# Attention with split operands: who rounds the turned queries and keys, who takes their rests, and when queries and keys are turned

## The reference, cut to what matters

```
scores = scale * q @ k.T                      # q, k, v: [4, 8, 576, 64] float32
thresh = max(scores, -1) - tau                # keep scores >= thresh, else -1e9
attn = softmax(scores);  x = attn @ v         # [2304, 512]
logits = x @ w_gate + modality_bias[id]       # top-1 of 8 experts, gate = its softmax
x = gate * (relu(x @ w1[e]) @ w2[e])          # w1 [8, 512, 1024]
h = x @ w_in;  out = (h * sigmoid(1.702 h)) @ w_out
```

## Time and profile before

| | us |
|---|---|
| median of 3 runs (lowest, highest) | 1011.82 (1011.54, 1012.12) |
| profiled execution, its own time | 1011.9 |
| its span | 1010.3 |
| PE / DVE / ACT / POOL busy | 967.1 / 530.6 / 432.4 / 286.2 |

### The profile page before, as it was taken

The page is one execution under the profiler, slowest core; times in us unless marked ns, Lnnn a source line. Parts: engine busy times, 40 slices in busy tenths (PEclk is TensorE's granted clock), DMA queues, the critical chain, the costliest instruction groups (busy, mean ns, idle before and its releaser), DMA issues.

```text
span 1010.3 us, 18677 instructions
## 1 busy us (share of the span) xinstructions
PE 967.1 (96%) x6365; PEld 853.6 (84%) x6366; DVE 530.6 (53%) x1138; ACT 432.4 (43%) x925; POOL 286.2 (28%) x357
## 2 busy tenths in 40 slices
PE   4999999999998899999999999999999999999996
PEld 4777777777676699999999999989999999999995
DVE  5998888999999875411124245522223223222221
ACT  3777787776667713312114254432222222222221
POOL 4766667676666503211112100010010000100101
PEclk8999999999999999999999999999999999999999
DMA  4334343334351506711110633110100100100000
GB/s 88 79 82 94 89 97 91 89 78 91 81 158 45 161 13 208 231 42 42 47 57 21 229 107 101 46 60 1 32 31 0 39 23 23 39 0 0 32 1 32
DMA packets 110669, 70.23 MB, mean 70 GB/s; under 512 B 87161, under 2 KB 95383, under 8 KB 110615
## 3 DMA queue, kind: packets, MB, share of 16 engines
q1 hardware_dynamic: 99959, 53.51, 20.3%
q0 software_dynamic: 4160, 10.51, 3.3%
q10 hardware_dynamic: 6496, 5.54, 1.7%
HBM read 45.68 MB, written 14.70 MB: 60 GB/s over the span
## 4 chain that ended last, share of the span: by engine, by line
PE 76%; DVE 12%; issue 7%; ACT 3%; DVEq 1%; DMA 0%; ACTq 0%; POOL 0%; POOLq 0%
PE s_ps L1842 19%; PE s_ps L1814 13%; PE s_ps L1687 11%; PE pt_ps L1814 6%; DVE probs L835 6%; PE misc L1762 5%; PE o_ps L1762 5%; PE s_ps L1620 5%; PE o_ps L1634 5%; PE pt_ps L1570 4%; DVE scores L1124 2%; ACT probs L1427 1%; PE pt_ps L1679 1%; PE pt_ps L1565 1%; DVE xs L844 1%
## 5 line engine op out<-in xcount | busy, mean ns | idle before, releaser
L1312 DVE TENSOR_TENSOR g<-s_ps,sig 128x384 f32<-128x384 f32 x96 | 53.5, 558 | 277.1 <-ACT sig L1537 277.1
L1537 ACT ACTIVATE sig<-s_ps 128x384 f32<-128x384 f32 x96 | 47.2, 491 | 271.5 <-PE s_ps L1842 271.5
L835 DVE SCALAR_TENSOR_TENSOR probs<-scores,thresh,probs 128x576 f32<-128x576 f32 x144 | 158.5, 1102 | 0.0
L790 POOL DMA_INDIRECT out_dram<-out_sb,table x18 | 17.8, 989 | 417.7 <-ACT out_sb L1512 414.7
L1124 DVE TENSOR_SCALAR_CACHE_REDUCE scores<-s_ps,taus 128x576 f32<-128x576 f32 x144 | 117.6, 817 | 31.2 <-PE s_ps L1620 11.4
L1427 ACT ACTIVATE probs<-scores,row_low 128x576 f32<-128x576 f32 x144 | 113.0, 785 | 45.4 <-DVE scores L1124 44.3
L1570 PE MATMUL pt_ps<-ident,probs 128*128 128x128 f32 x720 | 121.9, 280 | 10.7 <-ACT pT L1335 6.6
L1842 PE MATMUL s_ps<-yT_high,w_in_high 128*128 (+1 forms) x384 | 129.6, 337 | 0.3 <-issue 0.2
L1842 PE MATMUL s_ps<-yT_high,w_in_low 128*128 (+1 forms) x384 | 129.6, 338 | 0.0
L1842 PE MATMUL s_ps<-yT_low,w_in_high 128*128 (+1 forms) x384 | 129.1, 336 | 0.0
L1570 PEld LDWEIGHTS pt_ps<-ident,probs 128*128 128x128 f32 x720 | 83.3, 142 | 41.5 <-issue 25.5
(11 more groups left out here) (273 smaller groups left out, 2221.0 us busy)
## 6 DMA issues: line engine op xcount, KB each, us to landing
w_raw<-in_moe_w_dram SPq DMA_DIRECT2D x24, 512.0 KB, 4.5
yT_dram<-tile_yT ACTq DMA_DIRECT2D x10, 512.0 KB, 3.1
k_parts<-k_swap SPq DMA_DIRECT2D x31, 144.0 KB, 2.3
k_swap<-k_parts SPq DMA_DIRECT2D x31, 144.0 KB, 2.3
x_dram<-xs SPq DMA_DIRECT2D x32, 128.0 KB, 2.3
w_in_raw<-in_moe_w_in_dram SPq DMA_DIRECT2D x4, 1024.0 KB, 5.2
w_out_raw<-in_moe_w_out_dram SPq DMA_DIRECT2D x16, 256.0 KB, 2.7
qk<-in_k_dram SPq DMA_DIRECT2D x30, 128.0 KB, 2.4
```

Of the source, the lines that this page charges most:

```text
L835: dve.scalar_tensor_tensor(out=probs[:, i % PROB_SLOTS, 0:SEQ], in0=scores[:, i % SCORE_SLOTS], scalar=thresh[:, j, u:u + 1], in1=probs[:, ...
```

## The change

- GpSimd keeps only the threshold. ScalarE rounds: `round_both` (128 x 576: queries into the top of `q_parts`, keys into its bottom for a while) and `round_keys` (64 x 576 into the bottom of `k_swap`), side 0 after passes 3 and 4, side 1 after passes 5 and 7.
- VectorE takes both rests in one operation (`split_rests`, 128 x 576), in pass 4 after `write_x` (side 0) and in pass 7 (side 1). The rests land in `k_parts`, so the rest of the queries is in the wrong place.
- SyncE moves three things per side instead of two: the queries' rest and the keys' rest (`move_rests`), and, once the first has landed, the rounded keys (`move_keys`).
- SyncE's order in a pair p is now `move_rests` side 1 of p, `load_b` of p+2, `move_keys` side 1, `load_v`, `move_rests` side 0 of p+1, `store_x` of p-2, `move_keys` side 0, `load_a` of p+2.
- The nine tiles are turned in passes 0 to 4, two each but one in pass 2; TensorE waits for `load_b` in pass 3.
- The expert identifiers are loaded in pairs 2 to 5, not in the opening, and the bias of the rows is taken in quad 4. One early gather of rows moves from step 13 of the last quad to step 3.

```diff
-        TURN_TILES = {1: (0, 2), 3: (2, 4), 4: (4, 5), 6: (5, 7), 8: (7, 9)}
+        TURN_TILES = [(0, 2), (2, 4), (4, 5), (5, 7), (7, 9)]
@@ SyncE, load_a and load_b
-                    wait_apart(sp, turned, (quad * 2 + j - 1) * U)
+                    wait_apart(sp, turned, U if isinstance(quad, int) and quad * 2 + j == 2 else (quad * 2 + j - 2) * U + TPB)
-            def swap_keys(quad, j, side):
...
+            def move_rests(quad, j, side):
+                cols = K_COLS[side]
+                wait_apart(sp, split_low, (quad * 2 + j) * 2 + side)
+                sp.dma_start(q_parts[j][BOTTOM, Q_COLS[side]].bitcast(F32), k_parts[j][TOP, cols].bitcast(F32)
+                             ).then_inc(q_moved[side], 16)
+                sp.dma_start(k_swap[j][TOP, cols].bitcast(F32), k_parts[j][BOTTOM, cols].bitcast(F32)).then_inc(k_swapped[side], 16)
+            def move_keys(quad, j, side):
+                cols, pair = K_COLS[side], quad * 2 + j
+                wait_apart(sp, split_high, (pair * 2 + side) * 2)
+                wait_apart(sp, q_moved[side], (pair + side) * 16)
                 sp.dma_start(k_parts[j][TOP, cols].bitcast(F32), k_swap[j][BOTTOM, cols].bitcast(F32)).then_inc(k_swapped[side], 16)
@@ SyncE, step
+                    if on(pair, 1, PAIRS):
+                        move_rests(quad, j, 1)
                     if on(pair, 0, PAIRS - 2):
                         load_b(quad + 1, j)
-                    if on(pair, 0, PAIRS):
-                        swap_keys(quad, j, 1)
+                    if on(pair, 1, PAIRS):
+                        move_keys(quad, j, 1)
...
                     if on(pair, 0, PAIRS):
                         load_v(quad, j)
+                    if on(pair, 0, PAIRS - 1):
+                        move_rests(quad + j, 1 - j, 0)
+                    if on(pair, 2, PAIRS + 2):
+                        store_x(quad - 1, j)
+                    if on(pair, 0, PAIRS - 1):
+                        move_keys(quad + j, 1 - j, 0)
+                    if w1_pass:
+                        load_w1(first_expert_of(sp), 0, range(2, DB))
                     if on(pair, 0, PAIRS - 2):
                         load_a(quad + 1, j)
-                    if on(pair, 0, PAIRS - 1):
-                        swap_keys(quad + j, 1 - j, 0)
...
+                    if quad in (1, 2):
+                        load_ids(quad - 1, j)
@@ SyncE, opening: after load_b(0, 1)
+            move_rests(0, 0, 1)
             sp.dma_start(bias_sb[:], ...
...
-            for bp in range(BATCH // 2):        # eight loads of ids
...
+            move_keys(0, 0, 1)
             step(0)
@@ VectorE
+            def split_rests(pair, j, side):
+                cols = K_COLS[side]
+                wait(dve, split_high, (pair * 2 + side) * 2 - 1)
+                dve.tensor_tensor(k_parts[j][:, cols], qkT_raw[:, cols], q_parts[j][:, Q_COLS[side]].bitcast(F32), ALU.subtract
+                                  ).then_inc(split_low, 1)
...
+                    if u in (4, 7) and on(pair, 0, PAIRS - 1):
+                        split_rests(pair + 1, 1 - j, 0 if u == 4 else 1)
                     if on(n, 2, UNITS + 2):
                         mask(n - 2, (i - 2) % STEPS)
@@ ScalarE
+            def round_both(j, side):
+                act.copy(q_parts[j][:, Q_COLS[side]], qkT_raw[:, K_COLS[side]]).then_inc(split_high, 1)
+            def round_keys(j, side):
+                act.copy(k_swap[j][BOTTOM, K_COLS[side]], qkT_raw[BOTTOM, K_COLS[side]]).then_inc(split_high, 1)
...
+                    if u in (3, 4, 5, 7) and on(pair, 0, PAIRS - 1):
+                        side = 0 if u < 5 else 1
+                        if u in (3, 5):
+                            wait_apart(act, turned_copied, pair * U + U + (TAIL - 1 if side == 0 else TPB))
+                            round_both(1 - j, side)
+                        else:
+                            round_keys(1 - j, side)
@@ TensorE
-                if with_qk and tu in (0, TPB):
+                if with_qk and tu in (0, 3):
                     loaded, each = (qk_a_loaded, A_LOADS) if tu == 0 else (qk_b_loaded, B_LOADS)
                     wait(pe, loaded[1 - j], (quad + 1 + j) * each)
...
-                if with_qk:
-                    mm = transpose_qk(1 - j, tu, pt_ps[:, QK_AT + TURN_SLOT[tu]])
+                if with_qk and tu < TPB:
+                    first, end = TURN_TILES[tu]
+                    for tile in range(first, end):
+                        mm = transpose_qk(1 - j, tile, pt_ps[:, QK_AT + tile - first])
```

More of the change, by code:

```diff
@@ L285, in attention_moe_mlp_kernel @@
         k_swapped = [sem(f"k_swapped{side}") for side in range(2)]
+        q_moved = [sem(f"q_moved{side}") for side in range(2)]
         first_copied = sem("first_copied")
@@ L294, in attention_moe_mlp_kernel @@
         tau_ready = sem("tau_ready")
-        parts_ready = sem("parts_ready")
+        split_high = sem("split_high")
+        split_low = sem("split_low")
         scores_ready = sem("scores_ready")
@@ L414, in attention_moe_mlp_kernel @@
         TOP, BOTTOM = slice(0, DH), slice(DH, P)
-        TURN_SLOT = [0, 1] * (TPB // 2) + [0] + [0, 1] * (TAIL // 2)
-        TURN_TILES = {1: (0, 2), 3: (2, 4), 4: (4, 5), 6: (5, 7), 8: (7, 9)}
+        TURN_TILES = [(0, 2), (2, 4), (4, 5), (5, 7), (7, 9)]
         assert TPB == 5
@@ L480, in load_b @@
                              ).then_inc(qk_b_loaded[j], 16)
-            def swap_keys(quad, j, side):
-                split = (quad * 2 + j) * 8 + side * 4 - 4
+            def move_rests(quad, j, side):
                 cols = K_COLS[side]
-                wait_apart(sp, parts_ready, split + 1)
+                wait_apart(sp, split_low, (quad * 2 + j) * 2 + side)
[6 more added lines that the diff above has]
+                wait_apart(sp, q_moved[side], (pair + side) * 16)
                 sp.dma_start(k_parts[j][TOP, cols].bitcast(F32), k_swap[j][BOTTOM, cols].bitcast(F32)).then_inc(k_swapped[side], 16)
-                wait_apart(sp, parts_ready, split + 2)
-                sp.dma_start(k_swap[j][TOP, cols].bitcast(F32), k_parts[j][BOTTOM, cols].bitcast(F32)).then_inc(k_swapped[side], 16)
             def load_v(quad, j):
@@ L566, in early_part, with load_ids @@
                     sp.wait_ge(turned, UNITS)
-                    sp.wait_ge(parts_ready, PAIRS * 8 - 4)
+                    sp.wait_ge(split_high, (PAIRS * 2 - 1) * 2)
+                    sp.wait_ge(split_low, PAIRS * 2 - 1)
                     sp.wait_ge(order_stored, 16)
                     load_w2(first_expert_of(sp), 0)
+            def load_ids(bp, part):
+                at = bp * U
+                id_words = modality_id.bitcast(I32).rearrange("(b s w) -> b s w", b=BATCH, w=2)[:, :, 0]
+                ids_of = id_words[2 * bp + part]
+                rows, tail, cols = ((slice(0, LAST), SEQ - LAST, slice(at, at + TAIL)) if part == 0 else
+                                    (slice(LAST, P), SEQ - LAST, slice(at + TPB, at + U)))
+                sp.dma_start(ids[:, cols], ids_of[0:SEQ - LAST].rearrange("(t p) -> p t", p=P),
+                             allow_slow_non_contiguous=True).then_inc(routing_loaded, 16)
+                sp.dma_start(ids[rows, at + TAIL:at + TPB], ids_of[tail:].rearrange("(t p) -> p t", t=1),
+                             allow_slow_non_contiguous=True).then_inc(routing_loaded, 16)
             def first_expert_of(sp):
@@ L577, in step @@
                     pair = quad * 2 + j
+                    w1_pass = isinstance(quad, int) and (quad, j) == (QUADS - 2, 1)
+                    if on(pair, 1, PAIRS):
+                        move_rests(quad, j, 1)
                     if on(pair, 0, PAIRS - 2):
                         load_b(quad + 1, j)
-                    if on(pair, 0, PAIRS):
-                        swap_keys(quad, j, 1)
+                    if on(pair, 1, PAIRS):
+                        move_keys(quad, j, 1)
                     if isinstance(quad, int):
                         early_part(quad, j)
-                    if isinstance(quad, int) and (quad, j) == (QUADS - 2, 1):
+                    if w1_pass:
                         sp.wait_ge(first_expert_ready, 1)
@@ L612, in _ @@
                              w_gate.rearrange("(h p) e -> p h e", p=DH)).then_inc(gate_loaded, 16)
-            id_words = modality_id.bitcast(I32).rearrange("(b s w) -> b s w", b=BATCH, w=2)[:, :, 0]
-            for bp in range(BATCH // 2):
[L615 to L624, removed]
+            move_keys(0, 0, 1)
             step(0)
@@ L678, in _ @@
         def _(pool):
[L679 to L698, removed]
             pool.memset(ident[:], 0.0).then_inc(consts, 1)
@@ L719, in _ @@
                                pattern=[[1, P]], channel_multiplier=-1).then_inc(routing_consts, 1)
-            pool.wait_ge(routing_consts, 9)
-            split_keys(0, 0, 1)
-            split_queries(0, 0, 1)
             pool.wait_ge(tau_ready, 5)
@@ L736, in step @@
```

(25 more changed lines are left out.)

## The result

The changed kernel takes 1046.0 us (median of 4, 1041.8 to 1047.7) against 1011.9: a ratio of 1.033, 95% interval 1.031 to 1.035. It is slower, as forecast, but by 34 us and not by 16, and it lies outside the range. Its profiled execution took 1041.8, with a span of 1040.2 against 1010.3.

What follows compares the result with a forecast made beforehand. TensorE's own pace was taken to bound the loop (19.41 us a pair), with VectorE weighing most in later quads. Shifts from -3.5 in pair 0 to +17.8 at V(14), then +15.9, gave 1011.9 + 15.9 = 1028 us, range 1002 to 1040.

Steps and rivals of the forecast that it cites:

- Opening: Pair 0: with the identifiers' eight loads no longer ahead, TensorE resumes at 17.1 instead of 21.55, 4.5 us early.
- S: End of VectorE's rest in pass 4, which SyncE's moves, stores and loads wait for; 162.7 in pair 7's clock.
- V(1): First value matmul of pair 1, V(p) being that of pair p; forecast to shift by -3.5 us against before.
- The split's prices: ScalarE's rounding 0.67 us, VectorE's rest 0.75, its mask 0.82 instead of 1.05 in the loop and 1.14 later.
- The late load: Loop: load_a's sixth load lands 9.2 us behind S, 2.6 late for pass 0; period 21.7 us instead of 19.4.
- X to S: From pass 0's turning to the end of VectorE's rest in pass 4: 10.4 us of TensorE plus 2.0 of VectorE.
- the w1 term: Pair 13: two 512 KB loads of w1 stand ahead of load_a, +2.5 us, bounds 1 and 6.
- The tail: V(14) to attention's end: nothing more is loaded, VectorE is relieved by 1.4, then 0.5 us; shift +17.8 becomes +15.9.
- A: Rival: load_a is not on the path, TensorE keeps 19.4 us in the loop, later quads gain; 996 us, chance 0.13.
- B: Rival: as A, but ScalarE's roundings cost 0.5 us in each of seven loop periods; 1003 us, chance 0.06.
- C: Rival: SyncE's queue is crowded, the sixth load takes 0.9 us more in each of 13 periods; 1040 us, chance 0.15.
- D: Rival: GpSimd's threshold still stretches the mask, the load is only partly late, gain and loss cancel; 1012 us, chance 0.06.

## Why the prediction was wrong

- **Opening.** Forecast: TensorE resumes at 17.1. Measured: 17.14. X(1), pass 0 of pair 1, was forecast at 28.9 and came at 28.6. That is right partly by luck, as two errors cancel: the eight scores ran at the higher clock and S came at 19.97 instead of 20.9, and from S to X(1) took 8.7 instead of 8.0. V(1) came at 32.9 and not at 31.4, because the clock had fallen behind the stall.
- **The split's prices.** Forecast: rounding 0.67, rest 0.75, mask back at 0.82. Groups of the changed kernel, 60 to 200 us (busy, mean ns, idle before):
```profile
L1345 ACT CAST q_parts<-qkT_raw 128x576 fp32r<-128x576 f32 x12 | 8.2, 682 | 0.0
...
L815 DVE TENSOR_TENSOR k_parts<-qkT_raw,q_parts 128x576 fp32r<-128x576 f32 x12 | 9.0, 751 | 0.0
L824 DVE SCALAR_TENSOR_TENSOR probs<-scores,thresh,probs 128x576 f32<-128x576 f32 x54 | 43.9, 813 | 0.0
```
- **The late load.** Forecast: S to pass 0 is 9.3 us, the load 2.6 us late. Measured: 9.36 in pair 7, 9.5 on average over pairs 2 to 8, stalls mostly of 1.8 to 2.5. Right, and shown by moving load_a back, which takes away 46 us, the clock's share included.
- **X to S, the step that failed.** I put 12.4 us from pass 0's turning (X) to VectorE's rest (S), and took TensorE's 10.4 of it from a trace in which it never stood still. The cost of the lower clock behind a stall stood at nothing. In pair 5, where the clock did not fall, the sum comes out: from 120.83 to the end of this rest is 12.45 us.
```profile
132.53 0.75 DVE L815 TENSOR_TENSOR k_parts<-qkT_raw,q_parts 128x576 fp32r<-128x576 f32 x1
```
The four other pairs without a fall take 12.3 to 12.5. In pair 7, where it fell, it is 166.49 to 180.53, 14.0; the nine pairs with a fall take 13.8 to 15.2, together 16 us more than 9 x 12.4. So the whole miss of this step is the clock. I had seen the opening at half pace (0.44 a score matmul) and allowed for it there, but gave none of the 14 stalls that I forecast this consequence. The filled stall prices it at 15.3 us. With it the forecast of +16 would have been +31; 34 were measured.
- **What else was off.** Between V(2) and V(8) the changed kernel loses 23.2 us where 13.8 were forecast. Of the 9.4 more, 7.8 lie behind an X and are the lower clock, and 1.6 lie between S and X, which took 9.6 us on average and not 9.3. So even at the higher clock the period is not 21.7: from X(5) to X(6) it is 21.9, and 22.2 in the run with the stalls filled. V(13) to V(14) is 26.1, but 1.6 of it is the lower clock; the 24.5 that are left agree with the forecast 22.1 + 2.5, so the w1 term held. The tail gained more: V(14) to V(16) is 38.7 against 44.2, 5.5 us less where 1.9 were forecast; VectorE's relief was undersized (in V(14) to V(15) the mask took 1.21 us on average before and takes 0.81 now, and I had used 1.14). The tail pulls against the rest.
- **The rivals.** A was the mechanism of the unchanged order: it gave 996, and the kernel with load_a early takes 1000.3, 994.2 once ScalarE's rounding is moved. B was half right: with load_a early, ScalarE's rounding in pass 7 costs 0.3 us a period (19.8 against 19.5; not in passes 3 and 4, where I put it), but behind the late load it is hidden. C does not explain the miss: in the stalls of pairs 1 to 9 the sixth load landed in 1.9 to 2.2, and only two of the 14 took longer, 3.0 and 3.1. D is refuted: the mask is at 0.81 and the load fully late.
- **The range** reached 1040 by crowding of the queue alone. A stall on TensorE had to carry the lower clock as a term of its own, with both ends (0 and 14 x 1.6 = 22 us, by the price that pair 7 shows), and the range would have held the result.

What stays open: why the clock falls after one stall of about 2 us and not after the next. The traces show both, and no run here tells them apart.

## What to carry to other kernels

When an engine takes over work, follow the order of the queue that moves its results: an in-order queue turns every transfer behind a wait into part of that wait, also those, like the stores here, that do not need what is waited for. Put what the next pass needs ahead of the wait, and what nobody needs behind everything. And where a stall falls on TensorE, price it twice: the idle time, and the time at the lower clock behind it.

## What was not expected of the hardware

- Stalls of 1.8 to 2.5 us in a stream that otherwise keeps TensorE busy (20.4 of 23.0 us) were followed by the lower clock in 7 of 11 pairs of the profiled execution, and both longer ones (3.0 and 3.7 us) as well. In seven of these nine a fall cost 1.4 to 1.7 us from X to S, in the other two 2.3 and 2.8.
- A stall filled with 18 transposes of no use (2.1 us) costs less than the empty one: 1030.7 against 1046.0 us.
